# First attention unit with unsplit values, rests of the combined weight on GpSimd, one shift instruction per lane, and the opening of every engine in a written-out order

## The chip, the core and the metric

The kernel runs on one core of one Trainium2 chip. The metric is the device time of one execution in microseconds, the median of several runs. Engines are named as the profile names them: PE (TensorE), PEld (its weight loads), DVE (VectorE), ACT (ScalarE), POOL (GpSimd), SP (SyncE, which issues all DMAs here).

## What is computed

Attention with the 32 largest scores of each row kept, then a gated network, then a second network in which two products are multiplied and two weights follow each other:

```python
scores = scale * q @ k.T                       # 4 batches, 8 heads, 576 tokens, head size 64
kth = np.partition(scores, -32)[..., -32]      # the 32nd largest of each row
attn = softmax(where(scores >= kth, scores, -1e9))
x = concat_heads(attn @ v)                     # 2304 tokens x 512
h = x @ w_in                                   # 512 -> 2048
y = (h * sigmoid(h)) @ w_out                   # 2048 -> 512
out = ((y @ w1) * (y @ w2)) @ w3 @ w_out2      # 512 -> 1024 -> 1024 -> 512
```

## The kernel before

The 2304 tokens are 9 units of 256. Attention runs in 72 steps, step s being unit s // 8 and head s % 8; a step has two lanes of 128 queries, t = 2s and 2s + 1. The network of a unit (`H`, `Y`, then `A`, `B`, `O`) follows its eight attention steps, while the steps of the next unit run beside it.

Products are made in fp32r from split operands: x is rounded to x_hi, the rest x - x_hi is x_lo, and three products (hi·hi, hi·lo, lo·hi) are summed. ACT makes the rounded halves, POOL (or DVE) the rests. The names in the tables of order, by engine:

- PE: `QK` t (scores of a lane, L929), `T` t (transposes of its probabilities, L944 and L945), `PV` s (L965, nine products of 256 columns), `W34` m, part (w3 @ w_out2, computed on the chip in plain fp32, L977: 8 pieces m of 4 parts, two products of 512 columns each), `H`, `Y`, `A`, `B`, `O`.
- DVE: `TOP` (the 32 largest of a lane: four MAX8 at L828 and three MATCH_REPLACE at L830 for each lane, 14 instructions a step), `DEN`, `RDEN` (L837, L843, the sum of a row and its reciprocal), `LO` of even lanes (L848, L850), `XS` (L861, adds the two halves of PV), `W34` (L865, the rest of the combined weight, 128x512), `G`, `BM`, `X2`.
- ACT: `QR`, `KR`, `VR` (rounded q, k, v), `WS` (rounded weights, 16 chunks in two parts), `W12`, `W34`, `SC` (scores out of PSUM, L722), `MASK` (Prelu, L730), `EXP` (L738), `EV` (probabilities out of PSUM, L750 to L756), `XC`, `XH`, `TH`, `GR`.
- POOL: the rests to these (`QR` L600, `KR` L608, `VR` L614, `WS` L622, `W12` L629, `XL` L662, `GL` L668, `LO` of odd lanes L656), `BOUNDS` (L637 and L642, two short instructions for both lanes after the whole step's TOP), `NORM` (L649).
- SP: loads and stores. `RAW` and `WSK` load a chunk of w_in or w_out and store its split form; `WIN` and `WOUT` bring it back later, into rings of three places. `V`, `VS` load the values and store their split form, which the second unit that needs them loads back.

Each engine runs its own list in program order. The list is sorted by due times: a step's number plus a constant for the kind of work, from the table `LAG`, and for the network the positions that `mlp_positions` spreads from `M0` on. So an instruction that waits holds up all that stands behind it on its engine. PE can't start `H` of unit 0 before the x of steps 0 to 7 is split (`x_split`), nor `A` of unit 0 before all sixteen `W12` pieces are there (`w12_ready`). Seven chunks of w_in and w_out are split ahead of the network, the others just before PE takes them.

## Time and profile before

| | us |
|---|---|
| median of 3 runs (1113.38 to 1116.69) | 1113.53 |
| the profiled execution | 1112.51 |
| its span in the trace | 1110.7 |
| PE busy | 1048.4 (94%) |
| DVE busy | 931.9 (84%) |
| ACT busy | 775.7 (70%) |
| POOL busy | 619.6 (56%) |

The busy shares are means over stretches that differ: attention alone at the start, then network and attention together, and a last unit of network alone. The rows further down are therefore taken by stretch. The busy time of PE counts records whose ends are modelled; a plain fp32 product stands in the trace as two records (W34's 64 products are 128).

### The profile page before, as it was taken

To read this page: it belongs to the slowest core of one execution; us is meant where nothing else is said; L and a number is where in the kernel's file an instruction comes from. 1 tells how busy PE (TensorE), PEld (TensorE's weight loads), DVE (VectorE), ACT (ScalarE), POOL (GpSimd) and SP (SyncE) were. 2 spreads that over 40 slices of the span, in tenths; PEclk is the share of its full clock that TensorE was granted. 3 is DMA by queue.
4 is the path that set the end of the run, shared out by engine and by line. 5 is a ranking of instruction groups with operands and counts; after the bars stand their busy time and mean duration, and the time that the engine had idled before them with its cause. 6 is when DMAs were issued, how large, how long until landed. Compare 5 with 4: busy or idle time off the path is not lost.

```text
span 1110.7 us, 24334 instructions
## 1 busy us (share of the span) xinstructions
PE 1048.4 (94%) x7872; PEld 982.2 (88%) x7872; DVE 931.9 (84%) x2066; ACT 775.7 (70%) x1921; POOL 619.6 (56%) x803
## 2 busy tenths in 40 slices
PE   2998698999999999999999999999999999999998
PEld 1554598999999999999999999999999999999897
DVE  4999998989999999999998999999999999981110
ACT  3888888768776777787767776877677767774221
POOL 3777889666654555566544556665455445543211
PEclk9999599999999999999999999999999999999999
DMA  8998999969995898699858996999579748954962
GB/s 247 338 319 292 320 305 370 317 203 327 362 333 175 284 336 298 206 335 363 312 174 288 336 301 201 314 352 350 179 269 341 253 150 308 319 204 149 340 213 95
DMA packets 129053, 310.42 MB, mean 279 GB/s; under 512 B 14240, under 2 KB 43936, under 8 KB 128928
## 3 DMA queue, kind: packets, MB, share of 16 engines
q1 hardware_dynamic: 128928, 308.86, 80.6%
q8 instruction: 65, 1.06, 0.4%
q14 instruction: 60, 0.49, 0.1%
HBM read 263.19 MB, written 45.61 MB: 278 GB/s over the span
## 4 chain that ended last, share of the span: by engine, by line
PE 71%; DMA 11%; DVE 10%; issue 2%; ACT 2%; SPq 2%; POOL 1%; ACTq 0%; POOLq 0%; DVEq 0%
DMA win<-win_split 9%; PE ps_h L1033 6%; PE ps_h L1035 6%; PE ps_h L1034 6%; PE ps_s L929 5%; PE ps_x L965 5%; PE ps_h L995 5%; PE ps_y L1017 5%; PE ps_y L1019 5%; PE ps_y L1018 5%; PE ps_h L996 5%; PE ps_h L997 4%; DVE top L828 4%; PE ps_t L944 4%; PE ps_y L1046 3%; DVE rest L830 3%
## 5 line engine op out<-in xcount | busy, mean ns | idle before, releaser
L828 DVE MAX8 top<-rest 128x8 f32<-128x576 f32 x432 | 312.9, 747 | 0.0
L668 POOL TENSOR_TENSOR g_lo<-gate,g_hi 128x256 fp32r<-128x256 f32 x216 | 159.6, 739 | 181.8 <-ACT g_hi L796 180.3
L830 DVE MATCH_REPLACE8 rest<-top,rest 128x576 f32<-128x576 f32 x288 | 212.5, 743 | 0.5
L995 PE MATMUL ps_h<-x_hi,win 128*128 128x256 f32 x576 | 166.9, 290 | 12.7 <-DMA win<-win_split 12.7
L1033 PE MATMUL ps_h<-x_hi,w_hi 128*128 128x256 f32 x576 | 165.5, 287 | 4.5 <-DVE x_lo L884 4.5
L656 POOL TENSOR_TENSOR pT<-p_raw,pT 128x640 fp32r<-128x640 f32 x72 | 113.3, 1573 | 100.6 <-ACT pT L756 100.2
L1017 PE MATMUL ps_y<-g_hi,wout 128*128 128x256 f32 x576 | 164.9, 286 | 0.6 <-POOL g_lo L668 0.6
L1035 PE MATMUL ps_h<-x_hi,w_lo 128*128 128x256 f32 x576 | 162.7, 282 | 0.0
L1034 PE MATMUL ps_h<-x_lo,w_hi 128*128 128x256 f32 x576 | 162.7, 282 | 0.0
L996 PE MATMUL ps_h<-x_lo,win 128*128 128x256 f32 x576 | 162.1, 281 | 0.0
L997 PE MATMUL ps_h<-x_hi,win 128*128 128x256 f32 x576 | 162.0, 281 | 0.0
L1018 PE MATMUL ps_y<-g_lo,wout 128*128 128x256 f32 x576 | 161.6, 280 | 0.0
L1019 PE MATMUL ps_y<-g_hi,wout 128*128 128x256 f32 x576 | 161.6, 280 | 0.0
L649 POOL TENSOR_SCALAR probs<-probs,rden 128x576 f32<-128x576 f32 x144 | 107.6, 748 | 81.3 <-DVE rden L843 81.3
L796 ACT CAST g_hi<-gate 128x256 fp32r<-128x256 f32 x216 | 87.4, 405 | 83.3 <-DVE gate L871 52.5
L995 PEld LDWEIGHTS ps_h<-x_hi,win 128*128 128x128 f32 x576 | 109.1, 189 | 17.4 <-DMA win<-win_split 16.9
L730 ACT ACTIVATE probs<-scores,bounds 128x576 f32<-128x576 f32 x144 | 112.1, 779 | 14.1 <-POOL shift L642 14.1
L1033 PEld LDWEIGHTS ps_h<-x_hi,w_hi 128*128 128x128 f32 x576 | 109.8, 191 | 7.5 <-issue 6.3
L828 DVE MAX8 top<-scores 128x8 f32<-128x576 f32 x144 | 102.2, 751 | 16.7 <-ACT scores L722 15.5
L738 ACT ACTIVATE probs<-probs,shift 128x576 f32<-128x576 f32 x144 | 111.7, 777 | 0.0
L1034 PEld LDWEIGHTS ps_h<-x_lo,w_hi 128*128 128x128 f32 x576 | 109.8, 191 | 1.0
L1035 PEld LDWEIGHTS ps_h<-x_hi,w_lo 128*128 128x128 f32 x576 | 109.8, 191 | 0.0
(78 smaller groups left out, 2780.9 us busy)
## 6 DMA issues: line engine op xcount, KB each, us to landing
win<-win_split SPq DMA_DIRECT2D x135, 512.0 KB, 6.5
wout<-wout_split SPq DMA_DIRECT2D x135, 512.0 KB, 5.0
wout<-w_dram SPq DMA_DIRECT2D x72, 512.0 KB, 3.8
v_split<-v_dram SPq DMA_DIRECT2D x64, 320.0 KB, 5.6
k_split<-k_dram SPq DMA_DIRECT2D x64, 288.0 KB, 5.9
v_dram<-v_split SPq DMA_DIRECT2D x32, 320.0 KB, 6.0
k_raw<-kT SPq DMA_DIRECT2D x64, 144.0 KB, 5.1
k_dram<-k_split SPq DMA_DIRECT2D x32, 288.0 KB, 4.5
```

The source lines that it names most:

```text
L668: nc.gpsimd.tensor_tensor(g_lo[:, n % NR, :], gate[:, n % NG, :], g_hi[:, n % NR, :].bitcast(F32), ALU.subtract).then_inc(g_split, 1)
L828: nc.vector.max(best[:, 8 * n:8 * n + 8], sc if step == 0 else left).then_inc(topk_step, 1)
L830: nc.vector.match_replace(left, best[:, 8 * n:8 * n + 8], sc if step == 1 else left, BELOW_ALL).then_inc(topk_step, 1)
L995: nc.tensor.matmul(ps_h[:, f % 2, 0:UN], hi, xh, start=(c == 0), stop=False)
L996: nc.tensor.matmul(ps_h[:, f % 2, 0:UN], hi, xl, start=False, stop=False)
L997: m = nc.tensor.matmul(ps_h[:, f % 2, 0:UN], lo, xh, start=False, stop=(c == KC - 1))
L1017: nc.tensor.matmul(y, hi, gh, start=(f == 0 and d % 2 == 0), stop=False, skip_group_check=True)
L1018: nc.tensor.matmul(y, hi, gl, start=False, stop=False, skip_group_check=True)
L1019: m = nc.tensor.matmul(y, lo, gh, start=False, stop=(f == FC1 - 1), skip_group_check=True)
L1033: nc.tensor.matmul(ps_h[:, n % 2, 0:UN], hi, x2_hi[:, c, :], start=(c == 0), stop=False)
L1034: nc.tensor.matmul(ps_h[:, n % 2, 0:UN], hi, x2_lo[:, c, :], start=False, stop=False)
L1035: m = nc.tensor.matmul(ps_h[:, n % 2, 0:UN], lo, x2_hi[:, c, :], start=False, stop=(c == KC - 1))
```

## The change

It does five things.

1. Steps 0 to 7 (`FULL_STEPS`) keep probabilities and values unsplit. `EV` makes two copies into `p_full` (fp32), `PV` is five plain fp32 products of 256 columns straight from `v_raw`, and `XC` writes the finished x. In these steps `LO`, `XS` and `VR` are gone, from DVE, POOL and ACT. Unit 1, which uses the same values, loads them raw and splits and stores them (`FIRST_V`).
2. The rests of the combined weight go from DVE to POOL. POOL can't read PSUM, so ACT makes one more copy of 128x512 for each of the eight pieces (`w34_raw`). PE waits for the rounded half only.
3. `BOUNDS` (two instructions for both lanes) becomes `SHIFT`, one short instruction for each lane. `MASK` takes its bound from `top` itself and waits for the lane's own seven TOP instructions (`topk_step` is now one semaphore for each lane); only `EXP` waits for POOL.
4. The first 150 to 400 operations of every engine stand in a table, `FIRST_PLACES`; `in_order` sorts them by it and all later ones by due time.
5. `LAG`, `M0` and `TOP_SPAN` have new values, and `START_LAG` holds those of unit 0. w_out2 comes in four DMAs instead of two, and `H` waits for x piece by piece.

```diff
+FULL_STEPS = 8
-M0 = 9.882
+M0 = 9.846
-    "WIN": -0.143, "WOUT": -0.299, "OUT": 4.264, "QK0": -0.99, "QK1": -0.591, "T0": 1.468, "T1": 1.838,
+    "WIN": -0.443, "WOUT": -0.68, "OUT": 3.23, "QK0": -1.083, "QK1": -0.607, "T0": 1.354, "T1": 1.59,
+FIRST_PLACES = {
+    "tensor": {
+        "QK": (0, 2, 6, 8, 10, 12, 14, 20, 23, 28, 30, 37, 40, 43, 46, 51, 54, 59, 62, 67, 72, 76, 78,
...
+def in_order(engine, out):
...
+        if n < len(places) and places[n] >= 0:
+            first.append((places[n], op))
+        else:
+            rest.append((at, op))
+    return sorted(first, key=lambda o: o[0]) + sorted(rest, key=lambda o: o[0])
...
+                elif kind == "W34":
+                    m = op[1]
+                    pool.wait_ge(w34_rounded, m + 1)
+                    nc.gpsimd.tensor_tensor(w34[:, m % 2, 1, :], w34_raw[:, m % 2, :], w34[:, m % 2, 0, :].bitcast(F32),
+                                            ALU.subtract).then_inc(w34_split, 1)
...
+                elif kind == "SHIFT":
+                    t = op[1]
+                    pool.wait_ge(topk_step[t % 2], 7 * (t // 2) + 7)
+                    if t >= 4:
+                        pool.wait_ge(probs_ready, t - 3)
+                    nc.gpsimd.tensor_scalar(shift[:, t % 4, :], top[:, t % 4, TOPK - 1:TOPK], top[:, t % 4, 0:1], SCALE,
+                                            ALU.subtract, ALU.mult).then_inc(shift_ready, 1)
...
+                    nc.scalar.copy(w34_raw[:, m % 2, :], ps_y[:, m % 2, :])
                     nc.scalar.copy(w34[:, m % 2, 0, :], ps_y[:, m % 2, :]).then_inc(w34_rounded, 1)
...
-                    act.wait_ge(bias_ready, s + 1)
+                    act.wait_ge(topk_step[t % 2], 7 * (t // 2) + 7)
...
+                    if s < FULL_STEPS:
+                        nc.scalar.copy(p_full[0:D, 2 * KCH - 1, cols], tail(t))
+                        nc.scalar.copy(p_full[:, 0:KCH - 1, cols], ps_t[:, :, :]).then_inc(p_rounded, 1)
+                        continue
...
+                    if s < FULL_STEPS:
+                        pe.wait_ge(p_rounded, 2 * s + 2)
+                        pe.wait_ge(v_loaded[s % 2], 16 * (s // 2 + 1))
+                        for c in range(KCH):
+                            rows, at = (P, c) if c < KCH - 1 else (D, 2 * KCH - 1)
+                            m = nc.tensor.matmul(ps_x[0:D, 0:UN], v_raw[0:rows, s % 2, c, :], p_full[0:rows, at, :],
+                                                 start=(c == 0), stop=(c == KCH - 1))
+                        m.then_inc(pv_ready, 1)
+                        continue
...
-                    if f == 0:
-                        pe.wait_ge(x_split, KC * (u + 1))
...
+                        if f == 0:
+                            pe.wait_ge(x_split, KC * u + c + 1)
```

Three places show what the table does. The first is the start of PE's list. Before, the scores of the first four lanes come first:

```order
L929 MATMUL ps_s<-k_split,q_hi 128x288 x2
L929 MATMUL ps_s<-k_split,q_lo 128x288 x2
L929 MATMUL ps_s<-k_split,q_hi 128x288 x2
L929 MATMUL ps_s<-k_split,q_lo 128x288 x2
L929 MATMUL ps_s<-k_split,q_hi 128x288 x2
L929 MATMUL ps_s<-k_split,q_lo 128x288 x2
L929 MATMUL ps_s<-k_split,q_hi 128x288 x2
L929 MATMUL ps_s<-k_split,q_lo 128x288 x2
L977 MATMUL ps_y<-wo_sb,w3T_sb 128x512 x2
```

After (L1131 is QK, L1188 is W34):

```order
L1131 MATMUL ps_s<-k_split,q_hi 128x288 x2
L1131 MATMUL ps_s<-k_split,q_lo 128x288 x2
L1188 MATMUL ps_y<-wo_sb,w3T_sb 128x512 x2
L1131 MATMUL ps_s<-k_split,q_hi 128x288 x2
L1131 MATMUL ps_s<-k_split,q_lo 128x288 x2
L1188 MATMUL ps_y<-wo_sb,w3T_sb 128x512 x6
L1131 MATMUL ps_s<-k_split,q_hi 128x288 x2
L1131 MATMUL ps_s<-k_split,q_lo 128x288 x2
L1188 MATMUL ps_y<-wo_sb,w3T_sb 128x512 x2
L1131 MATMUL ps_s<-k_split,q_hi 128x288 x2
L1131 MATMUL ps_s<-k_split,q_lo 128x288 x2
```

Parts of W34 now stand between the scores: two products before lane 1, six before lane 2, and the first two of the second piece (which needs the second w3 load) before lane 3.

The second is DVE at the end of the opening. Before, from `LO` of lane 12 (step 6), which stands behind the whole of step 7, to `XS` of step 6, far into step 8:

```order
L848 TENSOR_TENSOR pT<-ps_t,pT 128x4x128
L850 TENSOR_TENSOR pT<-ps_x,pT 64x128
L865 TENSOR_TENSOR w<-ps_y,w 128x512
L828 MAX top<-scores 128x8 x2
L830 MATCH_REPLACE rest<-top,scores 128x576 x2
L828 MAX top<-rest 128x8 x2
L830 MATCH_REPLACE rest<-top,rest 128x576 x2
L828 MAX top<-rest 128x8
L837 TENSOR_SCALAR den_eps<-den 128x2
L843 RECIPROCAL rden<-den_eps 128x2
L828 MAX top<-rest 128x8
L861 TENSOR_TENSOR x_raw<-ps_x,x_raw 64x256
```

After, the end of step 8 and the start of step 9 (L1034 and L1036 are TOP, L1043 and L1050 are DEN and RDEN; the first RDEN shown is that of step 7, the second that of step 8):

```order
L1043 TENSOR_SCALAR den_eps<-den 128x2
L1036 MATCH_REPLACE rest<-top,rest 128x576 x2
L1034 MAX top<-rest 128x8 x2
L1050 RECIPROCAL rden<-den_eps 128x2
L1034 MAX top<-scores 128x8 x2
L1036 MATCH_REPLACE rest<-top,scores 128x576 x2
L1034 MAX top<-rest 128x8 x2
L1036 MATCH_REPLACE rest<-top,rest 128x576
L1043 TENSOR_SCALAR den_eps<-den 128x2
L1050 RECIPROCAL rden<-den_eps 128x2
L1036 MATCH_REPLACE rest<-top,rest 128x576
L1034 MAX top<-rest 128x8 x2
```

The three foreign operations are gone from the steps of unit 0, and the reciprocal of step 7 now comes right behind the last TOP of step 8.

The third is POOL from the last split of x of unit 0 (`XL` 3) on, which releases the network. Before:

```order
L662 TENSOR_TENSOR x_lo<-x_raw,x_hi 128x256
L637 TENSOR_SCALAR bounds<-top 128x4
L642 TENSOR_TENSOR shift<-bounds 128x2
L629 TENSOR_TENSOR w_lo<-o_sb,w_hi 128x512
L656 TENSOR_TENSOR pT<-p_raw,pT 128x5x128
L668 TENSOR_TENSOR g_lo<-gate,g_hi 128x256
```

After (L858 is XL, L824 W12, L838 SHIFT, L817 WS, L852 LO, L795 QR, L845 NORM, L864 GL):

```order
L858 TENSOR_TENSOR x_lo<-x_raw,x_hi 128x256
L824 TENSOR_TENSOR w_lo<-o_sb,w_hi 128x512 x2
L838 TENSOR_SCALAR shift<-top 128x1 x2
L817 TENSOR_TENSOR win<-w_raw,win 128x512
L852 TENSOR_TENSOR pT<-p_raw,pT 128x5x128
L795 TENSOR_TENSOR q_lo<-q_raw,q_hi 128x256
L824 TENSOR_TENSOR w_lo<-o_sb,w_hi 128x512 x2
L845 TENSOR_SCALAR probs<-probs,rden 128x576 x2
L864 TENSOR_TENSOR g_lo<-gate,g_hi 128x256 x2
```

More of the weight work (four W12 and one WS where one W12 stood) now lies between the release of the network and its first `GL`.

## Rows read from the trace of the kernel before

**Rows 1.** Windows: stretch; busy PE, PEld, DVE, ACT, POOL; granted clock, DMA share, GB/s.
```profile
7.00:29.00 22.00, 8.68 (x21) 5.44 (x21) 13.52 (x28) 7.35 (x14) 6.17 (x9) 1.00 1.02 290
29.00:107.00 78.00, 75.46 (x295) 43.77 (x293) 76.43 (x166) 64.47 (x149) 57.44 (x66) 1.00 0.97 324
107.00:136.00 29.00, 14.86 (x64) 12.46 (x65) 28.13 (x62) 23.86 (x55) 26.07 (x31) 0.59 0.90 298
136.00:206.00 70.00, 64.62 (x516) 62.89 (x514) 61.55 (x136) 58.59 (x144) 61.61 (x69) 0.98 0.97 337
206.00:1000.00 794.00, 782.65 (x6217) 761.33 (x6215) 737.15 (x1643) 588.99 (x1482) 439.53 (x591) 1.00 0.81 282
1000.00:1111.00 111.00, 102.13 (x768) 96.29 (x766) 15.15 (x36) 30.12 (x78) 25.86 (x34) 1.00 0.57 199
```

**Rows 2.** Timeline of PE: first product of H and of A, unit 0.
```profile
136.07 0.56 PE L995 MATMUL ps_h<-x_hi,win 128*128 128x256 f32 x1
...
206.66 0.35 PE L1033 MATMUL ps_h<-x_hi,w_hi 128*128 128x256 f32 x1 [0.42 <-DVE x_lo L884]
```

**Rows 3.** Timeline of DVE: where steps 0, 1, 2 and 10 begin.
```profile
16.25 0.76 DVE L828 MAX8 top<-scores 128x8 f32<-128x576 f32 x1 [1.31 <-ACT scores L722]
...
25.24 1.40 DVE L828 MAX8 top<-scores 128x8 f32<-128x576 f32 x2
...
36.94 1.42 DVE L828 MAX8 top<-scores 128x8 f32<-128x576 f32 x2
...
135.25 1.42 DVE L828 MAX8 top<-scores 128x8 f32<-128x576 f32 x2
```

**Rows 4.** Lines of DVE, 36.9 to 135.2 (busy, mean ns, idle before).
```profile
L865 DVE TENSOR_TENSOR w<-ps_y,w 128x512 fp32r<-128x512 f32 x8 | 5.5, 682 | 0.1
L848 DVE TENSOR_TENSOR pT<-ps_t,pT 128x512 fp32r<-128x512 f32 x8 | 5.4, 680 | 0.1
L861 DVE TENSOR_TENSOR x_raw<-ps_x,x_raw 64x256 f32<-64x256 f32 x8 | 3.4, 422 | 0.7 <-ACT x_raw L763 0.5
...
L850 DVE TENSOR_TENSOR pT<-ps_x,pT 64x128 fp32r<-64x128 f32 x9 | 2.6, 284 | 0.1
```

**Rows 5.** Timeline of SP and PE: the first w3 loads, W34 early and later.
```profile
16.95 6.33 SPq L540 DMA_DIRECT2D w3T_sb<-w3T  x3
...
25.55 3.75 PE L977 MATMUL ps_y<-wo_sb,w3T_sb 128*128 128x512 f32 x4 [5.86 <-DMA w3T_sb<-w3T]
...
30.06 3.61 PE L977 MATMUL ps_y<-wo_sb,w3T_sb 128*128 128x512 f32 x8
```

**Rows 6.** Timeline of PE at full clock: a PV and the product behind it.
```profile
142.40 1.23 PE L965 MATMUL ps_x<-pT,v_split 128*128 128x256 f32 x9
143.46 0.28 PE L1017 MATMUL ps_y<-g_hi,wout 128*128 128x256 f32 x1
```

**Rows 7.** Lines of POOL, 135 to 206.
```profile
L629 POOL TENSOR_TENSOR w_lo<-o_sb,w_hi 128x512 fp32r<-128x512 f32 x10 | 12.9, 1290 | 1.6 <-ACT w_hi L710 1.6
L668 POOL TENSOR_TENSOR g_lo<-gate,g_hi 128x256 fp32r<-128x256 f32 x16 | 11.8, 736 | 1.7 <-ACT g_hi L796 1.6
L656 POOL TENSOR_TENSOR pT<-p_raw,pT 128x640 fp32r<-128x640 f32 x5 | 7.8, 1562 | 2.3 <-ACT pT L756 2.3
...
L649 POOL TENSOR_SCALAR probs<-probs,rden 128x576 f32<-128x576 f32 x10 | 7.5, 747 | 2.2 <-DVE rden L843 2.2
```

**Rows 8.** Timeline of POOL: a VR of unit 0, XL 3 and the sixteenth W12.
```profile
38.17 0.87 POOL L614 TENSOR_TENSOR v_split<-v_raw,v_split 128x320 fp32r<-128x320 f32 x1 [2.35 <-ACT v_split L694]
...
134.49 0.73 POOL L662 TENSOR_TENSOR x_lo<-x_raw,x_hi 128x256 fp32r<-128x256 f32 x1
...
190.84 1.29 POOL L629 TENSOR_TENSOR w_lo<-o_sb,w_hi 128x512 fp32r<-128x512 f32 x1
```

**Rows 9.** Waits, 206 to the end: PE's for w_in, SP's own for w_out's places.
```profile
PE ps_h L995 <- DMA win<-win_split: 10.9, 15, 1.6
...
SPq L510 <- PE ps_y L1048: 288.2, 69, 7.7
```

More of the change, by code:

```diff
@@ L21 @@
 BELOW_ALL = -3.0e38
-STEEP = 1.0e30
+STEEP = 2.0 ** 90
 KC = DM // P
@@ new lines, in in_order, with lag @@
+def in_order(engine, out):
+    first, rest, seen = [], [], {}
+    for at, op in sorted(out, key=lambda o: o[1][1:]):
+        places = FIRST_PLACES.get(engine, {}).get(op[0], ())
+        n = seen[op[0]] = seen.get(op[0], -1) + 1
+        if n < len(places) and places[n] >= 0:
[3 more added lines that the diff above has]
+    return sorted(first, key=lambda o: o[0]) + sorted(rest, key=lambda o: o[0])
+def lag(kind, s):
+    return s + (START_LAG if s < H else LAG)[kind]
@@ L213, in split_steps @@
     for s in range(STEPS):
-        out.append((s + LAG[q], ("QR", s)))
-    for e, (s, _, _, _, fresh) in enumerate(ENTRIES):
-        if fresh:
-            out += [(s + LAG[k], ("KR", e)), (s + LAG[v], ("VR", e))]
+        out.append((lag(q, s), ("QR", s)))
+    for e, (s, _, _, _) in enumerate(ENTRIES):
+        if k_fresh(e):
+            out.append((lag(k, s), ("KR", e)))
+        if v_fresh(e):
+            out.append((lag(v, s), ("VR", e)))
     return out
@@ L224, in act_order @@
         for lane in range(2):
-            out += [(s + LAG[f"{kind}{lane}"], (kind, 2 * s + lane)) for kind in ("SC", "MASK", "EXP", "EV")]
-        out.append((s + LAG["XC"], ("XC", s)))
+            out += [(lag(f"{kind}{lane}", s), (kind, 2 * s + lane)) for kind in ("SC", "MASK", "EXP", "EV")]
+        out.append((lag("XC", s), ("XC", s)))
         if s % 2:
-            out.append((s + LAG["XH"], ("XH", s // 2)))
+            out.append((lag("XH", s), ("XH", s // 2)))
     for m in range(FC2):
@@ L248, in pool_order @@
         for lane in range(2):
-            out += [(s + LAG[f"{kind}{lane}"], (kind, 2 * s + lane)) for kind in ("NORM", "LO")]
-        out.append((s + LAG["BOUNDS"], ("BOUNDS", s)))
+            out += [(lag(f"{kind}{lane}", s), (kind, 2 * s + lane)) for kind in ("SHIFT", "NORM", "LO")[:2 if s < FULL_STEPS else 3]]
         if s % 2:
-            out.append((s + LAG["XL"], ("XL", s // 2)))
+            out.append((lag("XL", s), ("XL", s // 2)))
+    for m in range(FC2):
+        out.append((LAG["W34"] + LAG["W34_PACE"] * m + LAG["W34_LO"], ("W34", m)))
     for (kind, u, f), p in MLP_AT.items():
@@ L263, in dve_order @@
     for s in range(STEPS):
-        for step in range(7):
-            for lane in range(2):
-                out.append((s + TOP_SPAN * (2 * step + lane) / 14, ("TOP", s, step, lane)))
-        out += [(s + LAG[kind], (kind, s)) for kind in ("DEN", "RDEN", "XS")]
-        out += [(s + LAG["LOD"], ("LO", t)) for t in (2 * s, 2 * s + 1) if on_vector(t)]
-    for m in range(FC2):
-        out.append((LAG["W34"] + LAG["W34_PACE"] * m + LAG["W34_LO"], ("W34", m)))
+        for lane in range(2):
+            out += [(lag("TOP", s) + TOP_SPAN * (2 * step + lane) / 14, ("TOP", 2 * s + lane, step)) for step in range(7)]
+        out += [(lag(kind, s), (kind, s)) for kind in ("DEN", "RDEN")]
+        if s >= FULL_STEPS:
+            out += [(lag("XS", s), ("XS", s)), (lag("LOD", s), ("LO", 2 * s))]
     for (kind, u, f), p in MLP_AT.items():
```

300 lines of the change are left out of this document (177 added, 123 removed), and 101 rows, old and new, of tables (FIRST_PLACES, LAG, START_LAG).

## Prediction

> **What bounds the kernel now.** I read the windows first, cut where the work changes [rows 1]. From 206 us on PE is busy 782.65 of 794 us and then 102.13 of 111: the network and the later attention run at PE's pace, and 20.2 us of idle time are all that can be won there. Before 107 us both DVE (76.43 of 78) and PE (75.46 of 78, with W34 as its filling) are full. From 107 to 136 only DVE is (28.13 of 29); PE has run out of W34, is busy for 14.86 us and its granted clock falls to 0.59, near the 1.2 GHz level. From 136 to 206 everything is dense, POOL with 61.61 of 70 most of the helpers. So the end is a sum: the network starts at 136.07 with its first H, unit 0's second half (A) at 206.66 [rows 2], and from there 904 us of PE work follow. The change is worth what it moves these two points.
>
> **The opening on DVE.** One step of TOP alone is 14 instructions; from the second MAX8 of step 0 at 16.25 to step 1 at 25.24 there are 13, so 0.69 each and 9.7 a step [rows 3]. Steps 2 to 9 took 135.25 - 36.94 = 98.3 us, 12.3 each. In them stand, foreign to TOP, eight W34 rests (5.5), LO (5.4 + 2.6) and XS (3.4), 16.9 in all [rows 4]. The change takes all of them out. What is left is 98.3 - 16.9 = 81.4, or 10.2 a step; by the other way, 9.7 and some 0.3 for DEN and RDEN, it is 10.0. I take 10.0. The order also matters: before, H stands behind T 17, so behind ten full steps of TOP; now PV 7 needs RDEN 7, right behind step 8, thus nine.
>
> **The first steps.** Here the new order costs something. Lane 1's scores now stand behind W34's first two products, and lane 3's behind the first two of the second piece. Plain fp32 ran at 0.94 us a record (3.75 for 4) at first, against 0.45 later (3.61 for 8) [rows 5], so two products (four records) take 3.8 us early and 1.8 later. The first w3 and w_out2 loads are issued right behind the first k and q; together 1.5 MB, which at the 290 GB/s of rows 1 have landed by about 10 us. Lane 1's scores then reach DVE at about 15.5, hardly before the 16.25 of now. The second w3 load stands behind some 5.8 MB that are issued before it (the first w3 load, four w_out2 parts, four weight chunks, k, q, v and one store); with its own 0.5 MB, at 290 GB/s from about 3 us on, it lands at 24 to 27. Before, the first of these loads, issued at 16.95, reached PE at 25.55 [rows 5]. So lane 3 is ready at about 28, where TOP would want it at 25. Step 1 then ends at 28 + 13 x 0.69 = 37, about 1 us later than now, and step 8 at 37 + 7 x 10.0 = 107. With 2 us for mutual waits (the 2 to 3% that DVE and PE each lose in the stretch from 29 to 107) it is 109.
>
> **From there to the first H.** RDEN 7, two NORM (1.5 [rows 7]), transposes, two ACT copies, PV, copies of x, XL (0.73 [rows 8]). The PV of these steps is five fp32 products of 256 columns; a product of 512 is two records of 0.45 less their overlap, 0.86, so one of 256 is 0.43 and PV 2.15, against 1.06 for the nine of now (142.40 to 143.46) [rows 6]. For transposes, copies and handovers I put 3.5, bounded by 2 and 6 (one handover behind XL takes 134.49 + 0.73 to 136.07, 0.85 us). That makes 8, and H at 117.
>
> **The opening on PE**, which must agree. Now PE did, as time at full clock, 75.5 + 0.59 x 14.86 + 8.68 / 2 = 88.6 us of work before H [rows 1, 5]. The change adds 8 x 1.09 = 8.7 for PV and puts one T less before H: 96.8. By the second w3 load, at 26, PE can have done 8.5 of it; 26 + 88.3 = 114.3, and with 2.5 for waits 117. PE is as late as DVE, so this is a floor that the lighter DVE can't go below. Since PE stays full to the end, its clock should not fall before H. I take 117, with 111 and 122 as ends: the first with the second w3 load 3 us early and no waits, the second with three such stalls as lane 3's. **Gain at H: 19.**
>
> POOL takes over the eight W34 rests (1.29 each by the W12 row of the same size, 10.3) and loses eight VR (0.87 [rows 8]) and eight LO (1.56), 19.4: lighter by 9. Before H it was busy 89.7 of 129, so nothing of it shows here. ACT gains eight copies of 128x512 and loses more than these in EV and VR. Transfers were at 0.97 of their share and 324 GB/s from 29 to 107; the stores of seven v_split (0.32 MB each) go, and what is needed before H now has 19 us less. I cost it at nothing, as ends 0 to 5, within the 122. SHIFT for BOUNDS is the same busy time; that MASK no longer waits for POOL shortens a path that isn't last here.
>
> A rule speaks against the POOL part. The eight rests take 0.68 us on DVE and 1.29 for the same size on POOL [rows 4, 7]. The Trainium skill, GPSIMD Engine Reference, section 4.1 Engine selection, says to do two-input elementwise work on VectorE, since GpSimd is about twice as slow at it. The trace agrees on the ratio (1.9), but by that rule the move would be a loss of about 5 us, and it is one only if POOL is last; POOL's 39 idle us before H say it isn't.
>
> **From H to A**, POOL is last. Its list from XL 3 to the sixteenth W12, which A needs, took 192.1 - 134.5 = 57.6 us [rows 8], and A came 14 us later, so W12 had slack. In the new list the same piece holds four W12, one WS (1.29 each), four GL (0.74), three NORM (0.75), one LO (1.56), four VR (0.87, unit 1's values are split here now), one QR and one XL (0.73 each) more: 5.2 + 1.3 + 2.9 + 2.2 + 1.6 + 3.5 + 1.5 = 18.2. 57.6 + 18.2 = 75.8 from XL's start, 74 from H's; before, H to A was 70.6. **Cost: 3.5**, with 0 (PE's 64.6 busy us, POOL without waits) and 10 (POOL waiting as often as now in a fuller list) as ends. A is at 191.
>
> **From A on** PE's work is the same. The new LAG values move WIN and WOUT 0.3 and 0.38 of a step (some 4 and 5 us) ahead, against 10.9 us of waits for w_in [rows 9]; half of these could go, others come. I take 0, from -5 to +6.
>
> **Sum:** 1112.5 (the profiled execution) - 19 + 3.5 = 1097.0. The median stands 1.0 above that execution, so 1098.
>
> **The rivals.** *(a) Only DVE counts.* The second w3 load is in time, PE keeps up, H comes at 110 and A 70 us later, since POOL catches up before: -26, 1087. For it: DVE's 16.9 us and one step are certain. Against it: PE's 96.8 us. Chance 0.19. *(b) The opening stalls.* Two lists that are both full wait for each other, or transfers and SP's queue (three w3 loads held it for 6.33 us [rows 5], now four stand in a row) come late: H at 125, and 3.5 after it: -7.5, 1106. Chance 0.18. *(c) The gain is given back.* The network starts earlier but unit 1's x is not: DVE has only 6% less work than PE (737.15 of 782.65 [rows 1]), and the reserve built up by the late start is gone. Then H of unit 1 waits, and all but 1 or 2 us are lost: 1112. Against it: DVE stands nearly as far ahead of H as now (nine steps and a half against ten). Chance 0.07. *(d) Slower.* SP stands 288.2 us before the places of w_out [rows 9]; with WOUT and WIN further ahead in its list, k, v and the next WIN are queued behind that wait. A wait of PE for w_in is 10.9 / 15 = 0.73. If 43 of the 128 later chunks had to wait, that is 31.4 - 10.9 = 20.5 more, 1118; slower than now from 36 such waits on. Chance 0.06. The case that I forecast has 0.50.
>
> **How the numbers follow.** A measurement of this kernel tells 0.3% (3.3 us) from no change. Faster by more than that are the forecast, (a) and (b): 0.87. Within it is (c), 0.07; slower (d), 0.06. The range takes in the forecast's own ends, (a) and (b), 1086 to 1109, and leaves (c), (d) and a little of the others outside.
>
> **What would show it.** The first H of unit 0 at 117 (now 136.07) and A at 191 (206.66); lane 3's first MAX8 at 28; steps of TOP at 10.0 us; five fp32 products in 2.15 us; PE busy over 95% and a granted clock of 1.00 up to H; POOL over 90% busy from H to A; a distance from A to the end of 904. A first H before 112 shows the PE floor wrong, one after 122 shows more stalls; a distance from A to the end off by more than 6 shows that the new due times matter, which I have at nothing.

## The result, and the profile after

The changed kernel took 1106.27 us (median of 6 runs, 1104.69 to 1108.43), the kernel before in the same rounds 1113.45 (1110.83 to 1119.67): a ratio of 0.993, 95% interval 0.991 to 0.996. That is 7.2 us gained; the prediction said 15.5 (1098). Direction and range held, the size did not. Repeated twice, on other chips, the ratio was 0.993 (0.991 to 0.996) and 0.996 (0.994 to 0.998).

The profiled execution took 1104.69 us, its span is 1102.9. First the windows of the kernel after, cut at the same marks as [rows 1], with the first H and A as borders (busy PE, PEld, DVE, ACT, POOL; granted clock, DMA share, GB/s):

```profile
7.00:29.00 22.00, 15.63 (x36) 8.36 (x37) 10.87 (x22) 10.30 (x19) 11.41 (x12) 0.84 1.11 317
29.00:107.00 78.00, 76.96 (x300) 41.81 (x298) 76.39 (x166) 62.94 (x137) 57.17 (x67) 1.00 1.01 350
107.00:119.60 12.60, 10.62 (x52) 6.31 (x52) 12.43 (x30) 9.73 (x25) 8.81 (x11) 1.00 0.51 159
119.60:198.00 78.40, 68.08 (x532) 64.94 (x530) 73.64 (x158) 69.61 (x170) 74.02 (x84) 0.98 0.98 344
198.00:1102.90 904.90, 885.84 (x6968) 858.56 (x6967) 747.53 (x1662) 620.03 (x1548) 476.38 (x623) 1.00 0.80 271
```

The stretch with a granted clock of 0.59 ahead of H is gone: PE is now busy, at 1.00, from 29 us up to H (98.7% up to 107 us, 10.62 of the last 12.6). Instead, the stretch from 7 to 29 us is at 0.84, where it was at 1.00. The transfers went from a share of 0.97 and 324 GB/s to 1.01 and 350 between 29 and 107 us.

PE's timeline, with the scores of lane 2, a PV of five plain products with the product behind it, the first H, the first split PV and the first A (start, busy, instruction, idle before it and who ended that):

```profile
23.57 0.82 PE L1131 MATMUL ps_s<-k_split,q_hi 128*128 128x288 f32 x2 [5.32 <-POOL k_split L803]
...
107.14 2.51 PE L1158 MATMUL ps_x<-p_full,v_raw 128*64 128x256 f32 x10
109.58 0.53 PE L1131 MATMUL ps_s<-k_split,q_hi 128*128 128x288 f32 x2
...
119.62 0.36 PE L1206 MATMUL ps_h<-x_hi,win 128*128 128x256 f32 x1
...
123.11 0.27 PE L1147 MATMUL ps_x<-ident,probs 128*64 128x128 f32 x1
127.07 1.56 PE L1176 MATMUL ps_x<-pT,v_split 128*128 128x256 f32 x9 [3.69 <-POOL pT L852]
...
197.95 0.28 PE L1244 MATMUL ps_h<-x_hi,w_hi 128*128 128x256 f32 x1
```

DVE's timeline: lane 2, DEN 0, lane 3, the start of step 2, and RDEN 7, the last thing on DVE that H needs:

```profile
25.58 0.76 DVE L1034 MAX8 top<-scores 128x8 f32<-128x576 f32 x1 [2.69 <-ACT scores L919]
...
27.91 0.27 DVE L1043 TENSOR_SCALAR den_eps<-den 128x2 f32<-128x2 f32 x1 [1.57 <-ACT probs L934]
...
29.87 0.76 DVE L1034 MAX8 top<-scores 128x8 f32<-128x576 f32 x1 [1.69 <-ACT scores L919]
...
38.92 1.42 DVE L1034 MAX8 top<-scores 128x8 f32<-128x576 f32 x2
...
110.01 0.15 DVE L1050 RECIPROCAL rden<-den_eps 128x2 f32<-128x2 f32 x1
```

PE's waits of the kernel after, first from 119 to 198 us, then to 1110 (us in total, times, longest):

```profile
PE ps_x L1176 <- POOL pT L852: 5.0, 2, 3.7
PE ps_y L1228 <- POOL g_lo L864: 3.6, 4, 2.4
PE ps_t L1146 <- DVE pT L1057: 1.1, 1, 1.1
...
PE ps_h L1206 <- DMA win<-win_split: 7.2, 12, 1.1
PE ps_h L1244 <- DVE x_lo L1086: 4.1, 7, 1.5
```

Set beside [rows 2], the three distances whose sum is the span are:

| | before | after | difference | forecast |
|---|---|---|---|---|
| start to first H | 136.1 | 119.6 | -16.5 | -19 |
| H to A | 70.6 | 78.4 | +7.8 | +3.5 |
| A to the end | 904.0 | 904.9 | +0.9 | 0 |

Of the 7.7 us that the sum missed, 2.5 lie ahead of H, 4.3 between H and A, 0.9 behind A. The experiments ask of each what it is. Where they name a distance, it is read from the first product of H and of A in the run's own trace. One trace stands for one execution. In the eight traces whose lists ahead of H are those of the kernel after, H came at 119.4 to 121.9. In all traces that leave the stretch from H to A as it is, with whatever opening, that stretch took 78.0 to 80.7 us; the one other trace of the old order had 72.9 where the kernel before has 70.6. Smaller differences than these say nothing.

### The profile page after: what moved, and what is told of

The parts are those of the page before. It is cut to its first block, busy times and chain, and to the rows that moved or that the text cites. A ratio compares the mean times of both kernels' runs of the same rounds, so it can differ in the third digit from the quotient of the medians.

```text
span 1102.9 us, 24262 instructions
## 1 busy us (share of the span) xinstructions
PE 1057.1 (96%) x7880; PEld 980.0 (89%) x7880; DVE 920.9 (83%) x2034; ACT 775.0 (70%) x1897; POOL 630.2 (57%) x803
## 3 DMA queue, kind: packets, MB, share of 16 engines
q8 instruction: 65, 1.06, 0.4%
## 4 chain that ended last, share of the span: by engine, by line
PE 64%; DVE 13%; DMA 9%; ACT 5%; issue 4%; POOL 3%; SPq 2%; ACTq 0%; POOLq 0%; DVEq 0%
DMA win<-win_split 7%; PE ps_h L1244 6%; PE ps_h L1246 6%; PE ps_h L1245 6%; DVE top L1034 5%; PE ps_s L1131 4%; DVE rest L1036 4%; PE ps_x L1176 4%; PE ps_t L1146 4%; PE ps_y L1228 3%; PE ps_h L1206 3%; PE ps_y L1230 3%; PE ps_y L1229 3%; PE ps_h L1208 3%; PE ps_h L1207 3%
## 5 line engine op out<-in xcount | busy, mean ns | idle before, releaser
L1034 DVE MAX8 top<-rest 128x8 f32<-128x576 f32 x432 | 311.2, 750 | 0.0
L864 POOL TENSOR_TENSOR g_lo<-gate,g_hi 128x256 fp32r<-128x256 f32 x216 | 159.5, 739 | 224.5 <-ACT g_hi L1002 224.1
L1036 DVE MATCH_REPLACE8 rest<-top,rest 128x576 f32<-128x576 f32 x288 | 213.7, 745 | 0.4
L852 POOL TENSOR_TENSOR pT<-p_raw,pT 128x640 fp32r<-128x640 f32 x64 | 101.0, 1578 | 76.1 <-ACT pT L959 75.4
L845 POOL TENSOR_SCALAR probs<-probs,rden 128x576 f32<-128x576 f32 x144 | 108.0, 752 | 32.6 <-DVE rden L1050 32.5
L1034 DVE MAX8 top<-scores 128x8 f32<-128x576 f32 x144 | 103.8, 752 | 19.7 <-ACT scores L919 18.1
L926 ACT ACTIVATE probs<-scores,top 128x576 f32<-128x576 f32 x144 | 111.6, 780 | 7.1 <-DVE top L1034 7.1
L1228 PEld LDWEIGHTS ps_y<-g_hi,wout 128*128 128x128 f32 x576 | 108.5, 188 | 6.6 <-issue 3.9
```

The costliest lines, as they stand in the source:

```text
L864: nc.gpsimd.tensor_tensor(g_lo[:, n % NR, :], gate[:, n % NG, :], g_hi[:, n % NR, :].bitcast(F32), ALU.subtract).then_inc(g_split, 1)
L1034: nc.vector.max(best[:, 8 * n:8 * n + 8], sc if step == 0 else left).then_inc(topk_step[t % 2], 1)
L1036: nc.vector.match_replace(left, best[:, 8 * n:8 * n + 8], sc if step == 1 else left, BELOW_ALL).then_inc(topk_step[t % 2], 1)
L1228: nc.tensor.matmul(y, hi, gh, start=(f == 0 and d % 2 == 0), stop=False, skip_group_check=True)
```

## What holds the first H

My theory after the result was that PE's list and DVE's list are each a floor of the opening. To see it, one list at a time was made lighter.

**PV cut to two products** (steps 0 to 7):

```diff
-                        for c in range(KCH):
+                        for c in (0, KCH - 1):
```

> Left out: in each of the first eight attention steps, PV does only its first and its last product, not all five. PE has 8 x 3 x 0.5 = 12 us less to do before the first H; no other engine's list changes. After the change the first H came at 119.6 us. Theory (both full: PE's own work is a floor of the opening): steps of TOP get shorter than 10.06 us and the first H comes by 4 us or more earlier than only the shorter last PV explains, at 114 or before. Rival (only the list of DVE counts): steps stay at 10.0 to 10.1, RDEN 7 stays at 109 to 110, and H gains only the last PV's 1.5 us, 118.

**Top-k on half the scores** (steps 0 to 7):

```diff
+                    if t < 2 * FULL_STEPS:
+                        sc, left = scores[:, t % 4, 0:S // 2], rest[:, t % 2, 0:S // 2]
```

> Changed in the computation: in the first eight attention steps the top-k search (MAX8 and MATCH_REPLACE8) looks at 288 of 576 scores. DVE has about 8 x 14 x 0.3 = 34 us less to do before the first H; no other engine's list changes. Theory (PE's own work is a floor): PE had 15.63 us of work before 29 us and 77 after it, so H can come to some 113 to 117 us, and DVE is then idle for 25 us or more. Rival (only the list of DVE counts): H comes at 95 or before.

**Both cuts together:**

> The two cuts together: PV of the first eight steps does its first and last product of five (PE 12 us less), and the top-k search of these steps looks at 288 of 576 scores (DVE some 30 us less). With either cut alone the first H came at 119.6 and 121.3 us, after the change at 119.6. Theory (PE's list and DVE's list are each a floor by itself, at nearly the same height): with both lighter H comes at 110 us or before. Rival (a third thing sets the pace, above all the transfers, whose share from 29 to 107 us was 1.01 to 1.03 in each of them): H stays at 117 us or later, with PE and DVE both waiting.

For each of the three kernels in this order, the window from 29 to 107 us, RDEN 7 and the first H:

```profile
29.00:107.00 78.00, 72.15 (x263) 36.88 (x262) 74.58 (x167) 61.66 (x136) 56.79 (x67) 0.98 1.02 353
...
110.03 0.14 DVE L1050 RECIPROCAL rden<-den_eps 128x2 f32<-128x2 f32 x1
...
119.65 0.56 PE L1206 MATMUL ps_h<-x_hi,win 128*128 128x256 f32 x1
```

```profile
29.00:107.00 78.00, 75.98 (x296) 41.02 (x294) 46.84 (x166) 61.88 (x136) 56.67 (x67) 1.00 1.01 349
...
110.09 0.15 DVE L1052 RECIPROCAL rden<-den_eps 128x2 f32<-128x2 f32 x1
...
121.35 0.36 PE L1208 MATMUL ps_h<-x_hi,win 128*128 128x256 f32 x1
```

```profile
29.00:107.00 78.00, 73.24 (x278) 37.96 (x277) 52.34 (x179) 65.72 (x145) 59.65 (x72) 1.00 1.01 352
...
103.98 0.14 DVE L1052 RECIPROCAL rden<-den_eps 128x2 f32<-128x2 f32 x1
...
113.88 0.56 PE L1208 MATMUL ps_h<-x_hi,win 128*128 128x256 f32 x1
```

The totals were 1106.91, 1108.98 and 1100.81 us, one run each. With DVE 30 us lighter, H is no earlier: PE, still busy 75.98 of 78, with waits of 2.0 us in all, holds it. That was expected, though at 113 to 117, where it came at 121. With PE 5 us less busy in the window, H is no earlier either: DVE holds it. Here the expectation (114 or before) was a miss and its rival nearer. With both lighter H gains 5.7 us, less than half of what either cut takes away, and misses the 110. A cut alone can't tell a list from the transfers, which are the same in all three kernels; both cuts together can, since H moved. So both lists are floors, at the same height, and a third floor lies close below. What it might be shows in the transfers' share, 1.01 to 1.02 in all three.

**More transfers.** Behind each w3 load two idle copies of 256 KB:

```diff
+                    for n in range(2):
+                        sp.dma_start(spare[2 * op[1] + n], w_out[P * op[1]:P * op[1] + P, :]).then_inc(spared, 16)
```

> The kernel after with transfers that nobody needs: behind each of the eight w3 loads SP issues two copies of 256 KB within DRAM, 4 MB in all, six eighths of them before 30 us and the rest before some 70. Nothing else changes. Theory (transfers have room between 30 and 107 us, PE's and DVE's lists are the floors): first H 0 to 3 us later, from the opening alone. Rival (the transfers, at a share of 1.01, are a floor too): 4 MB at 350 GB/s are 12 us, and H comes 8 us or more later.

**Fewer transfers.** Half of w3 and of w_out2 is loaded:

```diff
-                    sp.dma_start(w3T_sb[:, :, cols],
-                                 w3T.rearrange("(g p) f -> p g f", p=P)[:, :, cols]).then_inc(w3_loaded[op[1]], 16)
+                    sp.dma_start(w3T_sb[:, 0:FC2 // 2, cols],
+                                 w3T.rearrange("(g p) f -> p g f", p=P)[:, 0:FC2 // 2, cols]).then_inc(w3_loaded[op[1]], 16)
-                elif kind == "WO2":
+                elif kind == "WO2" and op[1] < W34_PARTS // 2:
-  ... matmul(ps_y[:, m_ % 2, :], w3T_sb[:, g, P * m_:P * m_ + P], wo2_sb[:, g, :],
+  ... matmul(ps_y[:, m_ % 2, :], w3T_sb[:, g % (FC2 // 2), P * m_:P * m_ + P], wo2_sb[:, g % (FC2 // 2), :],
```

> Changed in the computation: only the first half of each w3 load and of w_out2 is loaded, and W34's products of the second half of the sum read the first half again (same number, same size). 3 MB less are transferred, six eighths of it before 30 us; all engines have the same work. Theory (the transfers hold the opening: RDEN 3 at 67.6 to 68.5 us in all kernels, 9 us more with 4 MB more): PE's stall ahead of QK 2 goes under 3 us, RDEN 3 comes at 65 us or before, first H at 114 to 117. Rival (PE's and DVE's lists hold it, more transfers only hurt because there was no room left): H at 118.5 to 120.

> The 3 MB less together with both cuts of before (PV with two products of five, top-k on 288 of 576 scores in the first eight steps). With both cuts and all transfers the first H came at 113.9 us and RDEN 3 at 66.7. Theory (transfers are the next floor below the two lists): H at 109 us or before, RDEN 3 at 62 or before. Rival (what is left is the chain of handovers and PE's own 92 us of work): H at 112 to 114.

The kernel with idle copies, then the one with fewer loads (window, wait ahead of lane 2's scores, RDEN 3, that is the reciprocal of step 3, first H), then the one with fewer loads and both cuts:

```profile
29.00:107.00 78.00, 74.01 (x277) 39.77 (x276) 68.70 (x153) 57.01 (x125) 54.48 (x63) 0.96 1.02 366
...
75.71 0.17 DVE L1055 RECIPROCAL rden<-den_eps 128x2 f32<-128x2 f32 x1
...
128.57 0.37 PE L1211 MATMUL ps_h<-x_hi,win 128*128 128x256 f32 x1
```

```profile
29.00:107.00 78.00, 77.16 (x301) 41.52 (x300) 77.84 (x171) 62.09 (x137) 56.52 (x69) 1.00 0.96 324
...
20.05 0.50 PE L1131 MATMUL ps_s<-k_split,q_hi 128*128 128x288 f32 x2 [2.59 <-POOL k_split L803]
...
64.71 0.17 DVE L1050 RECIPROCAL rden<-den_eps 128x2 f32<-128x2 f32 x1
...
115.21 0.37 PE L1206 MATMUL ps_h<-x_hi,win 128*128 128x256 f32 x1
```

```profile
59.47 0.17 DVE L1052 RECIPROCAL rden<-den_eps 128x2 f32<-128x2 f32 x1
...
105.99 0.56 PE L1208 MATMUL ps_h<-x_hi,win 128*128 128x256 f32 x1
```

4 MB more: H 9.0 us later, though nobody uses them, and a total of 1116.35. (PE's mean granted clock from 29 to 107 us was 0.96 there, not 1.00, so a part of the 9.0 us may be slower records.) 3 MB less: H 4.4 us earlier with the same work on all engines, total 1101.05 in its one run. With both cuts as well H comes at 106.0, 7.9 us before the 113.9 with all transfers, total 1093.42. So that the transfers have room, the theory of the first of these three runs and the rival of the other two, falls. The transfers are a floor, and they work in the first 70 us: RDEN 3 stood at 67.6 to 69.7 us in the fourteen traces that have the new opening and all its transfers alone (66.7 with both cuts), 7 us later with more bytes and 4 earlier with fewer. From RDEN 3 to RDEN 7 it then takes some 41 us, with fewer loads (64.7 to 105.6) and with either list light alone too, and 37 where both are light. The 4 us of the kernel with fewer loads are all there when step 2 begins (34.73, where the kernel after has 38.92).

The Trainium skill, Perfetto Trace Analysis, section Engine Utilization, gives about 435 GB/s as what a single active core's 16 DMA engines can move. By that figure, as an estimate, 350 GB/s would leave a fifth free. The runs decide otherwise for this mix of packets: at a share of 1.01 and 350 GB/s another 16 GB/s on the mean were all that the idle copies could add (384 GB/s from 50 to 75 us, where the kernel after has 370), and they pushed the rest back.

**Another order of the first 30 us.** If bytes can't be spared, can those that are waited for go first? Two tries:

```diff
 SP    -W3 0, WO2 0, WO2 1, Q1, WO2 2, V0, WO2 3, RAW x4, K1, Q2, K2, Q3, KS0, W3 1
       +W3 0, WO2 0, WO2 1, Q1, K1, WO2 2, WO2 3, W3 1, Q2, RAW x4, V0, K2, Q3, KS0
 PE    -QK0, W34 0,0, QK1, W34 0,1, 0,2, 0,3, QK2, W34 1,0, QK3
       +QK0, QK1, W34 0,0, 0,1, 0,2, QK2, W34 0,3, QK3, W34 1,0
```

> The kernel after with another order of its first 30 us: k of step 1, q of steps 1 and 2 and the second w3 load are issued ahead of the four weight chunks and v; ACT and POOL split k and q of step 1 and 2 ahead of the first four weight pieces; PE does the scores of lane 1 ahead of W34's first piece and those of lanes 2 and 3 inside and right behind it; DEN 0 stands five instructions later on DVE. All amounts are the same. Theory (the openings of both lists, 5.3 us of wait of PE and 4.6 us of DVE, are lost time that H pays): lane 3's first MAX8 at 24 to 26 us instead of 29.9, first H at 115 to 116, total 3 to 4 us less than the kernel after. Rival (the lists lose it again further on, since PE's work and the transfers stay the same): H at 118 to 120, total the same.

That kernel took 1107.53 us (10 runs), ratio 0.994 (0.992 to 0.997), H at 119.7: no gain over the kernel after. PE's wait had only moved:

```profile
25.44 0.82 PE L1123 MATMUL ps_s<-k_split,q_hi 128*128 128x288 f32 x2 [6.01 <-issue]
```

Lane 2's scores stood on ACT behind four weight pieces whose raw data now landed later. The second try copies them first, and takes the old due times behind unit 0:

```diff
 ACT   -... KR1, QR2, WS 0,0, 1,0, 0,1, 1,1, W34 0, KR2, MASK0, SC2, EXP0, MASK1, EXP1, SC3
       +... KR1, QR2, SC2, SC3, WS 0,0, 1,0, 0,1, 1,1, W34 0, KR2, MASK0, EXP0, MASK1, EXP1
```

> The old due times from unit 0's end on, and the opening with the order of the earlier try (k 1, q 1, q 2 and w3 1 issued early, their splits ahead of the weight pieces, lane 1's scores ahead of W34) with one thing more: ACT copies the scores of lanes 2 and 3 ahead of the first four weight pieces too. In the earlier try they stood behind the pieces, so that PE waited 6.0 us at 19.4 us in front of lane 3's scores and the PE floor was not moved. Theory (PE's own work is the floor, its stalls before 30 us are what can be won): PE's longest stall between 8 and 29 us under 3 us, first H at 116 to 117.5, total 3 us under that of the kernel with the old due times alone (1101.9), 1099. Rival (DVE's list, that has 72 us from RDEN 0 to RDEN 7 in every run, or the transfers, hold it): H at 119 to 121, total 1101 to 1103.

DVE's timeline of this kernel, the start of step 1 and RDEN 3:

```profile
21.81 1.41 DVE L1013 MAX8 top<-scores 128x8 f32<-128x576 f32 x2
...
68.23 0.17 DVE L1029 RECIPROCAL rden<-den_eps 128x2 f32<-128x2 f32 x1
```

Lane 2 starts 4 us and lane 3 some 7 us earlier, and by RDEN 3 nothing of it is left; H comes at 119.4, the rival's value. The wait that took its place is PE's for the k of step 2 (3.75 us at 27.9), which was now issued behind more bytes. It took 1103.65 us (8 runs, 1098.79 to 1109.64), ratio 0.990 (0.987 to 0.994). By the ratio it is the fastest version I ran that computes everything, but its distance to the next, the old due times alone (0.991, 0.988 to 0.994), is inside the spread of the runs.

## What lengthens H to A

The prediction had POOL last there, and its busy share (74.02 of 78.4, 94%) looks like it.

**Rests of w1 and w2 cut on POOL:**

```diff
-                    nc.gpsimd.tensor_tensor(lo[:, k, cols], o_sb[:, c % 2, :], hi[:, k, cols].bitcast(F32),
+                    few = slice(cols.start, cols.start + 64)
+                    nc.gpsimd.tensor_tensor(lo[:, k, few], o_sb[:, c % 2, 0:64], hi[:, k, few].bitcast(F32),
...
-  hi, lo = w_hi[:, c, P * f:P * f + P], w_lo[:, c, P * f:P * f + P]
+  hi = lo = w_hi[:, c, P * f:P * f + P]
```

> Changed in the computation: the rest of each of the 16 pieces of the combined weights w1 and w2 is made for 64 of 512 columns on POOL, and the products of A and B that should read the rests read the rounded weights again (same number, same size). POOL has 14 x 1.0 = 14 us less to do between the first H and A; PE, DVE and ACT have the same. After the change H to A took some 77 us. Theory (POOL is the last list there): H to A in 70 us or less, with POOL's busy share under 85%. Rival (DVE and the waits between the lists set it, POOL is just full as well): H to A in 75 to 77 us.

**Top-k of steps 10 to 13 on half the scores**, alone and with the cut on POOL:

> Changed in the computation: the top-k search of attention steps 10 to 13 (lanes 20 to 27) looks at 288 of 576 scores. DVE has 56 x 0.3 = 17 us less to do between the first H and A, all else is as in the kernel after. There DVE was busy 73.62 of 78.38 us, the fullest but for POOL (74.02). Theory (DVE is the last list there): H to A in 73 us or less. Rival (no single list: PE's order with its waits for handovers): 77 us or more.

> The same cut on DVE and the cut of the earlier run on POOL (rests of the 16 pieces of w1 and w2 for 64 of 512 columns, the products read the rounded weights instead). DVE has 17 us and POOL 14 us less to do between the first H and A. Theory (DVE and POOL hold each other up, so that neither cut alone shows): H to A in 71 us or less. Rival (PE's 67 to 68 busy us and its handovers): 75 to 77 us.

The window from H to A of these three kernels:

```profile
119.40:196.80 77.40, 66.57 (x531) 64.73 (x530) 73.17 (x156) 68.66 (x169) 61.44 (x84) 0.98 0.99 346
```

```profile
121.90:200.70 78.80, 69.21 (x532) 66.46 (x530) 57.20 (x155) 69.13 (x170) 73.79 (x84) 0.96 0.97 344
```

```profile
120.10:198.70 78.60, 68.11 (x532) 66.36 (x530) 58.22 (x156) 68.61 (x169) 61.45 (x84) 0.96 0.98 342
```

12 us off POOL, 16 off DVE, both at once: H to A stays at 77.4 to 78.8. My theory (POOL last), the next (DVE last) and the third (the two hold each other) all fall; the rival stands, PE's own order with its handovers, though by exclusion (totals 1103.18, 1106.55 and 1103.71, one run each): neither ACT (69.61 of 78.4 us) nor the transfers (a share of 0.98) were lightened in this stretch. Neither POOL's nor DVE's list was last, however full.

Counted on PE: before, 64.8 us busy of 70.6 (5.8 idle); after, 68.1 of 78.4 (10.3 idle). So 3.3 us are more work and 4.5 more idle time. Part of the work is moved, not added: T 17 stood ahead of the first H and T 27 behind A before, now both lie between; and QK 32, which stood behind A, has taken the place of QK 22 with twice its products (22 records with q_hi instead of 20). Summed from each record's start to the next one's, without the idle time, the transposes take 1.6 us more than before, the scores 1.5 more, and H, Y and PV together 0.1. A lower clock adds hardly anything: it is 0.89 from 121 to 136 us, behind the wait for LO 17, but the kernel before has the same 0.89 from 136.1 to 151 us, behind its idle time ahead of H.

That wait, 3.69 us, is the largest piece of idle time, and it is 3.69 or 3.70 in all sixteen other traces with the new opening that leave this place as it is, whatever was cut. A wait that no lighter engine shortens is a chain, not a queue: T 17 ends at 123.4, ACT copies it in five instructions up to 125.2, POOL makes its rest from 125.28 to 126.8, PV 8 starts at 127.07. Before, T 17 stood ahead of H 0,0 and the products of H filled that time. The new table puts it right ahead of PV 8.

It isn't the only one. The next longest wait of PE there is as constant, 2.34 or 2.35 us in all eighteen traces with the new opening:

```profile
167.19 0.36 PE L1228 MATMUL ps_y<-g_hi,wout 128*128 128x256 f32 x1 [2.35 <-POOL g_lo L864]
```

The Y ahead of it ends at 164.3. ACT then rounds a piece of w_out (from 164.38), which by the trace had waited for that Y, POOL makes its rest from 165.08 to 166.36, and only behind it, up to 167.04, the g_lo that PE waits for. Before, the longest wait for g_lo in this stretch was 0.6. The two waits are 6.0 of the 10.3 idle us, more than all the 5.8 of before. No run took the second one out.

**One H between T 17 and PV 8:**

```diff
 PE    -H 0,0, H 0,1, T17, PV8          ACT   -W12 3, MASK x2, WS, EV17
       +H 0,0, T17, H 0,1, PV8                +W12 3, EV17, MASK x2, WS
 POOL  -SHIFT18, SHIFT19, WS 10,0, LO17
       +LO17, SHIFT18, SHIFT19, WS 10,0
```

> The kernel after with three places exchanged where the network starts: T 17 ahead of H 0,1 on PE, EV 17 ahead of two MASK and a weight piece on ACT, LO 17 ahead of two SHIFT and a weight piece on POOL. After the change PE stood idle for 3.69 us at 123.4 us, for LO 17 in front of PV 8. Theory (this wait is part of the cost from H to A): the wait shrinks to 1.5 us or less, and A comes 2 us or more earlier after H than in the kernel after (78.4 us). Rival (the lists are so full that the wait comes back as others before A): 78 us again.

```profile
120.40:201.50 81.10, 70.28 (x531) 67.31 (x530) 72.70 (x155) 69.30 (x170) 73.90 (x84) 0.94 0.95 330
...
127.53 1.30 PE L1171 MATMUL ps_x<-pT,v_split 128*128 128x256 f32 x9 [2.25 <-POOL pT L847]
```

The wait shrinks by 1.44 us, the time of the one H now behind T 17, and yet H to A is 2.7 us longer than in the kernel after, and longer than in any trace that leaves the stretch alone (78.0 to 80.7). The time came back as other waits (2.1 us for q_lo, which stood at 0.3) and as busy time at a lower mean clock, 0.94. Total 1108.11 (10 runs), ratio 0.995 (0.993 to 0.997). So the cause of the 3.69 us is shown, but taking a part of it out by hand doesn't pay. A version of this stretch as short as the 70.6 us of before was not found, so that these chains cost what they measure is argued, not shown.

## What the new due times do behind A

**Old due times** (`LAG`, `M0`, `TOP_SPAN`) for all that the table doesn't place, run twice, each time beside others:

> The kernel after, but with the due times (LAG, M0, TOP_SPAN) of the kernel before for all that FIRST_PLACES doesn't place, that is from the end of unit 0 on; the opening is untouched. The distance from unit 0's x2_lo to the end was 904.9 us before and 906.9 after. Theory (the new due times cost 2 us): distance 905, total 1104 to 1105 where the kernel after has 1106.3. Rival (due times are not it: the reserve that the attention had on the network is smaller): distance 907 or more, total no better than 1106.

> The kernel after once more, unchanged, on the same chip as the others and in as many rounds as the kernel with the old due times. Theory (the new due times cost some us after A): its total is 3 to 5 us above the 1101.9 us of the kernel with the old due times, its distance from A to the end 904 to 906 us, where that kernel had 898.0. Rival (the difference was the spread from run to run): total 1102 to 1103, or distances from A to the end that spread as widely.

> The kernel with the old due times once more. Theory (the new due times cost some 3 to 4 us): median 1101 to 1103 us, at least 2.5 us under that of the kernel after in the same rounds, and its distance from A to the end 898 to 902 us. Rival (spread of runs): medians within 2 us of each other.

> The kernel after, unchanged, beside the one with the old due times. Theory: median 1105 to 1107 us, distance from A to the end 904 to 906 us. Rival: within 2 us of the other kernel's median.

The windows from A to the end, in this order: old due times, after, old due times, after. The first two are from different chips, the last two from one. The first, 898.0, lies below both values that were expected of it (905, and 907 or more).

```profile
199.20:1097.20 898.00, 883.32 (x6969) 858.23 (x6967) 745.38 (x1662) 614.62 (x1548) 476.06 (x623) 1.00 0.79 273
```

```profile
198.50:1104.60 906.10, 886.74 (x6968) 859.05 (x6967) 747.35 (x1662) 619.46 (x1548) 475.12 (x623) 1.00 0.79 270
```

```profile
198.80:1099.70 900.90, 885.48 (x6969) 858.67 (x6967) 745.16 (x1662) 614.23 (x1548) 474.72 (x623) 1.00 0.79 272
```

```profile
199.10:1107.80 908.70, 886.62 (x6969) 858.94 (x6967) 747.53 (x1662) 619.61 (x1548) 475.22 (x623) 1.00 0.80 270
```

The medians are 1101.88 and 1104.97 us with the old due times, 1106.27, 1105.62 and 1107.16 with the new. All runs taken together, 14 with the old have a mean of 1104.1 (spread 3.4), 24 with the new 1106.6 (1.8): 2.5 us apart, with an uncertainty of about 1.0. So the new due times probably cost 2 to 3 us, a little; but the second comparison, the one within a chip, gave 2.2 us, short of the 2.5 that my theory asked for, and a profile with the old ones and the other opening had 905.3 us. The 898.0 alone, from the fastest of six runs, would have put them 7 to 8 us apart.

**Old due times for SP alone:**

> The kernel after with the old due times for SP's kinds alone (Q, K, KB, V, VB, KS, VS, WIN, WOUT, OUT); all compute engines keep the new ones. With all old ones A to the end was 898.0 us, with all new ones 904.9 and 906.1. Theory (SP's queue, where WOUT and WIN come earlier and then hold up q and k, is what the new due times cost): 899 to 901 us. Rival (the places on PE and ACT cost it): 904 to 906 us.

```profile
200.90:1141.10 940.20, 899.10 (x6969) 871.31 (x6967) 747.67 (x1662) 618.65 (x1548) 474.85 (x623) 0.98 0.76 261
...
PE ps_h L1195 <- DMA win<-win_split: 23.7, 12, 3.9
PE ps_y L1217 <- DMA wout<-wout_split: 6.7, 5, 2.4
```

1143.74 us, ratio 1.026 (1.021 to 1.031). Both theories fall: the old places of SP don't fit the new ones of the engines. With PE's positions from one set and SP's from the other, weights come late (30.4 us of waits where the kernel after has 7.2), and PE's mean granted clock is 0.98 instead of 1.00. The opposite mix wasn't run, so which set is better for SP stays open.

**The short shift alone**, in the kernel before:

```diff
-                    act.wait_ge(bias_ready, s + 1)
+                    act.wait_ge(topk_step, 14 * s + 13 + lane)
...
-                         bias=bounds[:, s % 2, lane, 1:2], scale=SCALE, alpha=STEEP)
+                         bias=top[:, s % 2, lane, TOPK - 1:TOPK], scale=-1.0, alpha=1.0 / STEEP)
```

> The kernel before with one part of the change alone: MASK takes the 40th value itself as its bias and waits for TOP only, and the shift of EXP is one instruction a lane on POOL (two a step, where there were BOUNDS's two). Nothing else is changed, the due times and the order are the old ones. The kernel after with the old due times had 898.0 us from A to the end, 6 us less than the kernel before (904.0). Theory (the short shift brings these 6 us, since MASK and EXP come sooner): from A to the end 898 to 900 us, first H 0 to 1 us earlier, total 1107 to 1109. Rival (what brings them is the unit's other side, V and weights that the list-scheduled start leaves otherwise, or nothing in particular): 903 to 905 us from A to the end, total as before.

```profile
136.10:209.00 72.90, 65.27 (x516) 63.20 (x514) 61.93 (x136) 58.75 (x145) 61.95 (x69) 0.97 0.95 322
209.00:1112.70 903.70, 887.00 (x6980) 860.60 (x6980) 751.76 (x1678) 617.85 (x1557) 473.38 (x623) 1.00 0.79 272
```

1115.04 us against 1114.66, ratio 1.001 (0.998 to 1.004), H at 136.1: the total doesn't change, as the rival and the prediction had it. (The bias is the 32nd value of a row, `top[..., TOPK - 1]` with `TOPK` 32, not the 40th.)

## Why the prediction was off

**Right.** The mechanism ahead of H: the opening lost DVE's foreign work and one step, PE stayed full at a granted clock of 1.00 from 29 to 107 us, and H gained 16.5 us. The floor on PE was argued against the 26 us of the rival "only DVE counts", and the run with a light DVE shows it. The second w3 load was forecast at 24 to 27 us and was used at 24.7. From the start of step 2 to RDEN 7 the forecast had seven steps of 10.0 and 2 us of waits, 72 us; it took 71.1 (38.92 to 110.01). The single step from 38.92 to 48.98 took 10.06. RDEN 7 was forecast with 109 and stands at 110.0. The shift cost nothing, as costed. That the rests on POOL cost nothing either is argued only, since no run has them on DVE: POOL was idle for 20.8 of the 78 us from 29 to 107, and PE waited for it 0.7 us there. By the rule of the Trainium skill, GPSIMD Engine Reference, section 4.1 Engine selection, that the prediction cites, the move would have been a loss. The trace agrees that POOL takes about twice as long; no run here shows a loss or a gain from it. The run with 12 us less on POOL bears on the stretch behind H alone, where these rests no longer are. A to the end, at nothing with -5 to +6, was +0.9.

**H, 119.6 instead of 117: two terms mis-sized, one dismissed.** By the forecast's own marks the 2.6 us are +1.9 up to step 2 (38.92, not 37), -0.9 for the steps and +1.6 from RDEN 7 to H (9.6, not 8). Lane 3 came at 29.87, not 28: PE waited 5.32 us for the k of step 1, which SP issued behind four weight chunks. I had costed that order for the w3 load alone. PV took 2.44 us to the next product's start, not 2.15: I took 0.43 a product from W34's overlap, and five such products take 0.49 each, 8 x 0.29 = 2.3 us more on PE. And the transfers "at nothing, as ends 0 to 5" are worth 4.4 us at 3 MB. At 1.01 the kernel after is shown to be held by them; that the share of 0.97 before was already a full queue is inferred from it, since no run lightens the transfers of the kernel before. A shorter opening with the same bytes had to meet this bound. That is a step that failed in kind. The row was there, and I read it as company, not as a bound.

**H to A, +7.8 instead of +3.5: the wrong engine.** This is the largest part of the miss, 4.3 of 7.7 us, and the step that failed is "POOL is last". It came from adding up POOL's list from XL 3 to the sixteenth W12: 75.8 forecast, 73.9 measured (120.00 to 193.9). The sum was good and bound nothing: A came 4 us after the last W12, and 12 us off POOL brought 1.0, which is inside the spread of the traces. What the runs show in its place is PE's own list: two T more and one lane's scores with twice the products (together most of the 3.3 us of work), and 4.5 us more of idle time, with two waits of constant length, 3.69 and 2.35 us, in it. Which T, QK and PV stand between H and A, and what fills the time of a handover, could be read from the two orders; I had costed the move of T 17 only where it helped, ahead of H.

**From the sum to the median.** The forecast missed the gain by 8.3 us, the distances by 7.7. The other 0.6 is that the median of the kernel after stands 1.6 above its profiled execution, not 1.0.

**Rivals.** (a), H at 110, did not come. (b), "the opening stalls", 1106, hit the number by luck, half by another way: it had H at 125 and 3.5 behind it. (c), gain given back between units, did not come: of 8.7 us at A 7.8 are left at the end. (d) did not come; PE's waits for w_in fell from 10.9 to 7.2 us.
